# First four pairs' quotient with tokens in partitions: one denominator a token, turned back by TensorE into the first chunk's input

## The chip, the cores and the metric

One core of a Trainium2 chip runs the kernel. The metric is the device time of one execution in microseconds (us); of the kernel before, three runs gave 948.98, 949.53 and 950.82, so the median is 949.53 us. TensorE does matrix products into PSUM, ScalarE (ACT) and VectorE (DVE) do the element-wise work, GpSimd (POOL) does element-wise work between SBUF tiles, and SyncE (SP) issues most of the loads.

## The reference

```python
def phi(x):                                        # x: q or k, times D ** -0.25
    proj = np.einsum('bhsd,md->bhsm', x, omega)
    h = proj - np.sum(x * x, axis=-1, keepdims=True) / 2.0
    return np.exp(h - np.max(h, axis=-1, keepdims=True)) / np.sqrt(m)
kv = np.einsum('bhsm,bhsd->bhmd', k_p, v)
z = np.sum(k_p, axis=2)
num = np.einsum('bhsm,bhmd->bhsd', q_p, kv)
den = np.einsum('bhsm,bhm->bhs', q_p, z)[..., None] + 1e-06
attn_out = num / den
...
h = x @ w_in;  g = h * np.clip(h + 3.0, 0.0, 6.0) / 6.0;  x = g @ w_out
h = x @ w_in2; g = h / (1.0 + np.exp(-1.702 * h));        out = g @ w_out2
```

There are 4 batches of 8 heads with 576 tokens and head size 64, 128 features, and two layers of width 512 with 2048 hidden units over the 2304 tokens. All is float32. The denominator is one number for each token and head.

## The kernel before

The 32 heads are taken as 16 pairs. A pair fills the 128 partitions with two heads' 64 dimensions, and its 576 tokens are four tiles of 128 and a tail of 64 (`ST`, `TAIL`). The five first pairs (`LEAD` = 5, numbers 0 to 4) are computed in a first stage, since the first chunk of 512 tokens of the layers needs four pairs (`PPB` = 4, one batch). Chunk 0 then starts, and the other eleven pairs are spread by a table of slots (`slot_units`) through the layers' products, where TensorE always has work.

For a pair the steps are these. `projection` (L479, L486) makes the features' exponents in PSUM. VectorE takes the row maxima (L866, L863) and from them and the norms two small operations (L878, L881: `h_max` and `bias`), `statistics` in all, once each for queries, keys and tail. ScalarE takes the exponentials (L685, L679). TensorE turns the queries' tiles (`turn`, L506) and ScalarE copies them out (L691), so that features lie in partitions. `key_values` (L516 to L522) multiplies keys with the values and a column of ones. VectorE copies the result into `state` (`keep`, L899 to L901); the sum of the keys is spread there over 64 columns. `numerator` (L542 in pairs 0 to 3, L553 later) then gives numerators and denominators with dimensions in partitions, in halves of 288 tokens. ScalarE copies the denominators out (L695), VectorE takes their reciprocal (L906) and multiplies (L910) into `X`.

The layers run in float32r with a high and a low part of every operand: ScalarE rounds `X` to `x_hi` (L739) and the low part `x_lo` is the difference, by GpSimd for the first three pairs (L398) and by VectorE for the fourth (L930). `hidden` (L585, L586, L591) makes the hidden blocks and `output` (L610 to L612) the second product. Block 0 of chunk 0 is done in four parts, one for each pair, inside the first stage; the layers' unbroken work begins with hidden block 1. GpSimd rounds and splits the first three pairs of weight blocks (`early_high` L412, `early_part` L403) and folds the squared rows of pairs 2 to 4 into norms (`fold_rows`, L378 and L380), all in the first stage. ScalarE squares the rows (L668).

Each engine has its own program in one fixed order, written out by hand at the ends of the engine blocks; engines wait for one another by counting semaphores. PSUM has eight banks: four for the projections of queries and keys (`acc`), one for hidden blocks and tails, and three (`att`) for turning, key-values and numerators.

## Time and profile before

| | before |
|---|---|
| median of three runs | 949.53 us |
| the profiled execution | 950.23 us |
| its span, first to last instruction | 947.9 us |
| TensorE busy | 934.7 us (99%) |
| VectorE busy | 402.7 us (42%) |
| ScalarE busy | 383.5 us (40%) |
| GpSimd busy | 174.1 us (18%) |

The span is the profiled execution without 2.3 us around it. TensorE is busy nearly all the time, so the end moves when TensorE's work changes, when it gets its work later, or when its clock changes. The shares are means over a first stage and the long remainder, and are to be read stage by stage.

### The profile page before, as it was taken

The numbers are of one execution on the slowest core, as the hardware profiler recorded it, in microseconds if no ns is written. First come the engines' busy times: TensorE is split into PE (matmuls) and PEld (weight loads), VectorE is DVE, ScalarE is ACT, GpSimd is POOL, SyncE is SP. The second block draws the span as 40 slices with busy tenths as digits, with TensorE's granted clock in tenths as the row PEclk, the third lists the DMA queues.
The fourth block names the chain that finished last, engine by engine and source line by source line (L and its number), as shares of the span: only waits on it lengthen the run. The fifth ranks groups of instructions, "written<-read, shape, count | busy, mean of one in ns | idle before, by whom it ended". The sixth has DMA issues, their size and how long they took to land.

```text
span 947.9 us, 12947 instructions
## 1 busy us (share of the span) xinstructions
PE 934.7 (99%) x5098; PEld 778.4 (82%) x5098; DVE 402.7 (42%) x708; ACT 383.5 (40%) x879; POOL 174.1 (18%) x185
## 2 busy tenths in 40 slices
PE   8899999999999999999999999999999999999998
PEld 6668788878888778888889988888888888888898
DVE  6866655655446553452223442233223222422332
ACT  7756555554445544442225652232223222322322
POOL 2575566121221120000004830000000000000000
PEclk9999999999999999999999999999999999999999
DMA  9434442111121211010002610001001000100010
GB/s 279 124 94 133 124 133 63 57 45 39 50 63 39 63 26 38 1 45 0 1 1 82 179 52 1 1 1 45 1 1 45 1 0 1 45 1 1 5 41 23
DMA packets 40731, 45.98 MB, mean 49 GB/s; under 512 B 21600, under 2 KB 22240, under 8 KB 40672
## 3 DMA queue, kind: packets, MB, share of 16 engines
q1 hardware_dynamic: 40304, 44.54, 15.6%
q8 instruction: 40, 0.66, 0.3%
q10 hardware_dynamic: 368, 0.62, 0.2%
q14 instruction: 19, 0.16, 0.1%
HBM read 40.44 MB, written 4.72 MB: 48 GB/s over the span
## 4 chain that ended last, share of the span: by engine, by line
PE 94%; DVE 4%; ACT 1%; issue 0%; DVEq 0%
PE acc L610 14%; PE acc L611 14%; PE acc L612 14%; PE hid L585 11%; PE hid L591 10%; PE hid L586 10%; PE att L585 4%; PE att L586 4%; PE att L591 4%; PE att L486 3%; PE att L553 2%; PE att L522 2%; PE att L506 1%; DVE row_max L866 1%; PE att L479 1%; DVE k_phi_b L906 1%
## 5 line engine op out<-in xcount | busy, mean ns | idle before, releaser
L610 PE MATMUL acc<-g_hi,w_out_hi 128*128 128x512 f32 (+1 forms) x640 | 241.5, 377 | 0.0
L612 PE MATMUL acc<-g_hi,w_out_lo 128*128 128x512 f32 (+1 forms) x640 | 236.0, 369 | 0.0
L611 PE MATMUL acc<-g_lo,w_out_hi 128*128 128x512 f32 (+1 forms) x640 | 235.9, 369 | 0.0
L585 PE MATMUL hid<-x_hi,w_in_hi 128*128 128x512 f32 (+1 forms) x476 | 181.7, 382 | 1.7 <-ACT x_hi L739 1.7
L591 PE MATMUL hid<-x_lo,w_in_hi 128*128 128x512 f32 (+1 forms) x476 | 176.2, 370 | 0.3 <-DVE x_lo L930 0.3
L586 PE MATMUL hid<-x_hi,w_in_lo 128*128 128x512 f32 (+1 forms) x476 | 175.5, 369 | 0.0
L945 DVE TENSOR_TENSOR g_lo<-R,g_hi 128x512 fp32r<-128x512 f32 (+1 forms) x160 | 106.9, 668 | 91.0 <-ACT g_hi L756 91.0
L610 PEld LDWEIGHTS acc<-g_hi,w_out_hi 128*128 128x128 f32 x640 | 120.8, 189 | 21.3 <-issue 1.9
L612 PEld LDWEIGHTS acc<-g_hi,w_out_lo 128*128 128x128 f32 x640 | 120.7, 189 | 20.5
L611 PEld LDWEIGHTS acc<-g_lo,w_out_hi 128*128 128x128 f32 x640 | 120.8, 189 | 19.3
L756 ACT ACTIVATE g_hi<-R 128x512 fp32r<-128x512 f32 (+1 forms) x160 | 94.6, 591 | 85.7 <-DVE R L940 52.6
L585 PEld LDWEIGHTS hid<-x_hi,w_in_hi 128*128 128x128 f32 x476 | 89.8, 189 | 19.7 <-issue 2.3
L938 DVE SCALAR_TENSOR_TENSOR R<-R,hid 128x512 f32<-128x512 f32 (+1 forms) x79 | 49.9, 631 | 129.2 <-ACT R L747 129.2
L591 PEld LDWEIGHTS hid<-x_lo,w_in_hi 128*128 128x128 f32 x476 | 89.7, 188 | 16.8 <-DVE x_lo L930 1.1
L586 PEld LDWEIGHTS hid<-x_hi,w_in_lo 128*128 128x128 f32 x476 | 89.9, 189 | 14.3
L747 ACT ACTIVATE R<-hid 128x512 f32<-128x512 f32 (+1 forms) x79 | 43.9, 556 | 106.0 <-PE hid L591 105.9
L940 DVE TENSOR_TENSOR R<-R,hid 128x512 f32<-128x512 f32 (+1 forms) x40 | 25.4, 634 | 113.5 <-ACT R L749 113.5
L940 DVE TENSOR_TENSOR R<-R,att 128x512 f32<-128x512 f32 (+1 forms) x40 | 25.4, 634 | 113.0 <-ACT R L749 113.0
L906 DVE RECIPROCAL k_phi<-k_phi 128x288 f32<-128x288 f32 x28 | 54.5, 1948 | 38.9 <-ACT k_phi L702 38.9
L749 ACT ACTIVATE R<-att 128x512 f32<-128x512 f32 (+1 forms) x40 | 22.2, 555 | 116.9 <-PE att L591 116.4
L749 ACT ACTIVATE R<-hid 128x512 f32<-128x512 f32 (+1 forms) x40 | 22.2, 555 | 116.2 <-PE hid L591 116.2
L585 PE MATMUL att<-x_hi,w_in_hi 128*128 128x512 f32 (+1 forms) x164 | 61.1, 372 | 0.0
(132 smaller groups left out, 1044.8 us busy)
## 6 DMA issues: line engine op xcount, KB each, us to landing
X<-w_in SPq DMA_DIRECT2D x16, 256.0 KB, 2.6
X<-w_out SPq DMA_DIRECT2D x16, 256.0 KB, 2.8
out_t<-X SPq DMA_DIRECT2D x16, 256.0 KB, 2.3
q_cols<-q_t SPq DMA_DIRECT2D x14, 288.0 KB, 2.8
k_cols<-k_t SPq DMA_DIRECT2D x14, 288.0 KB, 3.3
rows<-q_n SPq DMA_DIRECT2D x13, 288.0 KB, 3.5
rows<-k_n SPq DMA_DIRECT2D x13, 288.0 KB, 3.1
v_rows<-v_n SPq DMA_DIRECT2D x14, 256.0 KB, 3.3
```

Source lines behind the costliest of these rows:

```text
L585: nc.tensor.matmul(bank, w_hi[0][:, at], x_hi[:, k, x0:x0 + t], start=(k == 0), stop=False)
L586: nc.tensor.matmul(bank, w_lo[0][:, at], x_hi[:, k, x0:x0 + t], start=False, stop=False)
L591: last = nc.tensor.matmul(bank, w_hi[0][:, at], x_lo[:, k, x0:x0 + t], start=False, stop=(k == KC - 1))
L610: nc.tensor.matmul(bank, w_hi[1][:, at], g_hi[:, g, 0:t], start=(s == 0), stop=False)
L611: nc.tensor.matmul(bank, w_hi[1][:, at], g_lo[:, g, 0:t], start=False, stop=False)
L612: last = nc.tensor.matmul(bank, w_lo[1][:, at], g_hi[:, g, 0:t], start=False, stop=(s == J - 1))
L749: nc.scalar.activation(R[:, 0:t], h, ACT.Sigmoid, scale=1.702).then_inc(gate_ready, 1)
L756: nc.scalar.activation(g_hi[:, n % G_SLOTS, 0:t], R[:, 0:t], ACT.Copy).then_inc(g_hi_ready, 1)
L906: nc.vector.reciprocal(d, d).then_inc(recip_done, 1)
L938: nc.vector.scalar_tensor_tensor(out=r, in0=r, scalar=6.0, in1=h, op0=ALU.min, op1=ALU.mult).then_inc(gated, 1)
L940: nc.vector.tensor_tensor(r, r, h, ALU.mult).then_inc(gated, 1)
L945: nc.vector.tensor_tensor(g_lo[:, n % G_SLOTS, 0:t], R[:, 0:t], g_hi[:, n % G_SLOTS, 0:t].bitcast(F32), ALU.subtract).then_inc(g_ready, 1)
```

## The change

In pairs 0 to 3 the quotient is computed with tokens in partitions. `keep` copies key-values and the keys' sum as they are, 65 columns for a head. `quotient` on TensorE uses the turned queries as the stationary operand and these 65 columns as the moving one, once for a tile of 128 tokens and head, and the tail's tile against both heads. The 65th column is the denominator. VectorE adds the epsilon to nine columns of denominators, takes one reciprocal of 128x9, and multiplies by it into a tile by tokens (`xs`, named x_by_token). TensorE turns that back (`turn_back`), four tiles and the tail. ScalarE rounds the four tiles from PSUM straight to `x_hi`; VectorE copies only the tail's 64 tokens to `X` and takes `x_lo` from PSUM. The denominators' copies on ScalarE, the copies by halves, and GpSimd's three `x_lo` go. Two of ScalarE's squares come earlier, the others after the turned queries. GpSimd folds and splits in another order. The diff, cut to its core:

```diff
@@ keep @@
-                if by_columns(a):
-                    ones, values = state[:, 2:4, :], state[:, 0:2, :]
...
+                if by_token(a):
+                    nc.vector.tensor_copy(state[:].rearrange("p c d -> p (c d)")[:, 0:2 * (D + 1)],
+                                          bank[:, P:P + 2 * (D + 1)]).then_inc(state_ready, 1)
+                    nc.vector.tensor_copy(tile_of(a, KQ, 0, ST), bank[:, 0:P]).then_inc(tails_out, 1)
+                    return
@@ TensorE @@
+            def quotient(a):
+
+                q, sums = q_turned(a), state[:].rearrange("p c d -> p (c d)")[:, 0:2 * (D + 1)]
...
+                if a > 0:
+                    pe.wait_ge(x_ready, a)
+                for h in range(2):
+                    for t in range(ST):
+                        last = nc.tensor.matmul(num_bank(a, h)[:, t * (D + 1):(t + 1) * (D + 1)], q[:, h, t * P:(t + 1) * P],
+                                                sums[:, h * (D + 1):(h + 1) * (D + 1)], start=True, stop=True)
+                    if h == 0:
+                        last = nc.tensor.matmul(num_bank(a, 0)[:, ST * (D + 1):(ST + 2) * (D + 1)], tile_of(a, KQ, 0, ST), sums,
+                                                start=True, stop=True)
+                    last.then_inc(nd_done, 2)
+
+            def turn_back(a):
+                pe.wait_ge(xs_ready, a + 1)
+                for t in range(ST):
+                    nc.tensor.transpose(back_bank(a)[:, t * P:(t + 1) * P], xs[:, t, :], ident[:])
+                nc.tensor.transpose(num_bank(a, 0)[:, 0:P], xs[:, ST, :], ident[:]).then_inc(xs_turned, 1)
@@ turn @@
                 if 0 < a < LEAD and h == 0:
-                    pe.wait_ge(den_ready, dens_to(a - 1, 1))
+                    pe.wait_ge(xs_ready, a)
                 elif 0 < a < LEAD:
-                    pe.wait_ge(x_written, 2 * (a - 1) + 1)
+                    pe.wait_ge(x_written, 2 * (a - 1) + 2)
@@ ScalarE @@
+            def first_high(a):
+
+                act.wait_ge(xs_turned, a + 1)
+                nc.scalar.activation(x_hi[:, a, 0:ST * P], back_bank(a)[:, 0:ST * P], ACT.Copy).then_inc(x_hi_ready, 1)
@@ VectorE @@
+            def quotient(a):
+                tiles = [num_bank(a, h)[:, 0:ST * (D + 1)].rearrange("p (t c) -> p t c", t=ST) for h in range(2)]
+                dve.wait_ge(nd_done, 4 * a + 2)
+                nc.vector.tensor_scalar(dens[:, 0:ST], tiles[0][:, :, D], EPS, None, ALU.add)
+                for h in range(2):
+                    rows_h, _, den = tail_of(h)
+                    nc.vector.tensor_scalar(dens[rows_h, 2 * ST:GROUPS], num_bank(a, 0)[rows_h, den], EPS, None, ALU.add)
+                dve.wait_ge(nd_done, 4 * a + 4)
+                nc.vector.tensor_scalar(dens[:, ST:2 * ST], tiles[1][:, :, D], EPS, None, ALU.add).then_inc(dens_set, 1)
+                dve.wait_ge(dens_set, a + 1)
+                nc.vector.reciprocal(dens[:], dens[:]).then_inc(dens_ready, 1)
...
+                    nc.vector.tensor_tensor(xs[:, 0:ST, h * D:(h + 1) * D], tiles[h][:, :, 0:D],
+                                            dens[:, h * ST:(h + 1) * ST].unsqueeze(2).to_broadcast([P, ST, D]), ALU.mult)
...
+            def take_back(a):
+
+                dve.wait_ge(xs_turned, a + 1)
+                for h in range(2):
+                    rows_h = slice(h * D, (h + 1) * D)
+                    nc.vector.tensor_copy(x_at(a, ST * P, TAIL, h * D, (h + 1) * D), num_bank(a, 0)[rows_h, rows_h]).then_inc(x_written, 1)
+                dve.wait_ge(x_hi_ready, a + 1)
+                nc.vector.tensor_tensor(x_lo[:, a, 0:ST * P], back_bank(a)[:, 0:ST * P], x_hi[:, a, 0:ST * P].bitcast(F32),
+                                        ALU.subtract).then_inc(x_ready, 1)
@@ order of VectorE @@
                 keep(a)
                 statistics(a + 1, "k")
                 statistics(a + 1, "tail")
-                normalise(a, 0)
-                normalise(a, 1)
-                if a + 2 < LEAD - 1:
-                    statistics(a + 2, "q")
+                quotient(a)
+                statistics(a + 2, "q")
+                take_back(a)
@@ order of GpSimd @@
+            for a in (2, 3, 4):
+                fold_rows(a)
+                for r in (2 * a - 4, 2 * a - 3):
+                    early_high(r)
+                    early_part(r)
```

On TensorE the part from the numerators of pair 1 to the key-values of pair 2 stands in the kernel before as follows (`att` and `acc` are PSUM banks, `hid` the bank of the tails):

```order
L542 MATMUL att<-q_phi_b,state 64x288 x4
L486 MATMUL acc<-omega,X 128x128 x8
L542 MATMUL att<-q_phi_b,state 64x288 x4
L506 MATMUL att<-ident,q_phi 128x128 x4
L486 MATMUL acc<-omega,X 128x128 x8
L506 MATMUL att<-ident,q_phi 128x128 x4
L516 MATMUL att<-ident,q_tail_phi 128x128
```

In the changed kernel TensorE has at the same place:

```order
L523 MATMUL att<-state,q_phi_b 128x65 x4
L526 MATMUL att<-state,q_tail_phi_b 128x130
L523 MATMUL att<-state,q_phi_b 128x65 x4
L475 MATMUL acc<-omega,X 128x128 x8
L495 MATMUL att<-ident,q_phi 128x128 x4
L533 MATMUL att<-ident,x_by_token 128x128 x4
L534 MATMUL att<-ident,x_by_token 128x128
L475 MATMUL acc<-omega,X 128x128 x8
L495 MATMUL att<-ident,q_phi 128x128 x4
L503 MATMUL att<-ident,q_tail_phi 128x128
```

The second half of the quotient now stands ahead of the next projection, and five turns back stand between the two turns of the next pair's queries.

VectorE has, from the tail's statistics to the copy of the next pair's key-values, in the kernel before:

```order
L881 SCALAR_TENSOR_TENSOR bias<-h_max,half_norm 128x2
L906 RECIPROCAL k_phi_b<-k_phi_b 128x288
L910 TENSOR_TENSOR X<-att,k_phi_b 128x288
L906 RECIPROCAL k_phi_b<-k_phi_b 128x288
L910 TENSOR_TENSOR X<-att,k_phi_b 128x288
L866 TENSOR_REDUCE row_max<-acc 128x4 x2
L878 SCALAR_TENSOR_TENSOR h_max<-row_max,half_norm 128x8
L881 SCALAR_TENSOR_TENSOR bias<-h_max,half_norm 128x8
L899 COPY state<-att 128x128
```

and in the changed kernel:

```order
L899 TENSOR_SCALAR dens<-att 128x4
L902 TENSOR_SCALAR dens<-att 64x1 x2
L904 TENSOR_SCALAR dens<-att 128x4
L906 RECIPROCAL dens<-dens 128x9
L912 TENSOR_TENSOR x_by_token<-att,dens 128x4x64
L914 TENSOR_TENSOR x_by_token<-att,dens 64x64
L912 TENSOR_TENSOR x_by_token<-att,dens 128x4x64
L914 TENSOR_TENSOR x_by_token<-att,dens 64x64
L850 TENSOR_REDUCE row_max<-acc 128x4 x2
L865 SCALAR_TENSOR_TENSOR h_max<-row_max,half_norm 128x8
L868 SCALAR_TENSOR_TENSOR bias<-h_max,half_norm 128x8
L923 COPY X<-att 64x64 x2
```

The statistics of the next queries (L850 to L868) now stand between the quotient and the copies out of the turned-back tail; `x_lo` (L925) follows the copies.

GpSimd has in the kernel before, from the fold of pair 3 to that of pair 4:

```order
L378 TENSOR_TENSOR X<-X 128x18x32
L378 TENSOR_TENSOR X<-X 128x18x16
L378 TENSOR_TENSOR X<-X 128x18x8
L378 TENSOR_TENSOR X<-X 128x18x4
L378 TENSOR_TENSOR X<-X 128x18x2
L380 TENSOR_TENSOR half_norm<-X 128x18
L403 TENSOR_TENSOR w_out_lo<-X,w_out_hi 128x512
L412 CAST w_in_hi<-X 128x512
L412 CAST w_out_hi<-X 128x512
```

and in the changed kernel, for pair 2 and again for 3 and 4:

```order
L390 TENSOR_TENSOR rows<-rows 128x18x32
L390 TENSOR_TENSOR rows<-rows 128x18x16
L390 TENSOR_TENSOR rows<-rows 128x18x8
L390 TENSOR_TENSOR rows<-rows 128x18x4
L390 TENSOR_TENSOR rows<-rows 128x18x2
L392 TENSOR_TENSOR half_norm<-rows 128x18
L419 CAST w_in_hi<-X 128x512
L410 TENSOR_TENSOR w_in_lo<-X,w_in_hi 128x512
L419 CAST w_out_hi<-X 128x512
L410 TENSOR_TENSOR w_out_lo<-X,w_out_hi 128x512
```

Four operations on weights now stand behind every fold. In the kernel before, four stood ahead of the first fold, three behind each of the first two, and three `x_lo` and two more behind the last.

## Rows read from the trace of the kernel before

**Rows 1.** Windows: us, busy (count) of PE, PEld, DVE, ACT, POOL, PEclk, DMA, GB/s.

```profile
0.00:57.63 57.63, 47.63 (x418) 35.99 (x418) 45.14 (x99) 39.39 (x114) 25.81 (x39) 0.99 0.62 186
57.63:947.90 890.27, 887.05 (x4682) 742.37 (x4680) 357.58 (x610) 344.08 (x765) 148.32 (x146) 1.00 0.13 40
```

**Rows 2.** Timeline, VectorE, pair 2: start, length in us, line, output<-input, count.

```profile
37.58 0.28 DVE L899 COPY state<-att 128x128 f32<-128x128 f32 x1
...
38.18 1.28 DVE L866 TENSOR_REDUCE row_max<-acc 128x4 f32<-128x512 f32 x2
...
39.85 0.42 DVE L863 TENSOR_REDUCE row_max<-hid 128x2 f32<-128x256 f32 x1
...
40.65 1.95 DVE L906 RECIPROCAL k_phi<-k_phi 128x288 f32<-128x288 f32 x1
42.70 0.46 DVE L910 TENSOR_TENSOR X<-att,k_phi 128x288 f32<-128x288 f32 x1
43.07 1.95 DVE L906 RECIPROCAL k_phi<-k_phi 128x288 f32<-128x288 f32 x1
...
47.68 0.29 DVE L899 COPY state<-att 128x128 f32<-128x128 f32 x1 [2.10 <-PE att L522]
```

**Rows 3.** Timeline, TensorE, pair 2.

```profile
33.72 1.16 PE L486 MATMUL acc<-omega,X 64*128 64x128 f32 x16 [0.41 <-ACT k_phi L685]
34.82 0.66 PE L506 MATMUL att<-ident,q_phi 128*128 128x128 f32 x4
35.31 0.27 PE L516 MATMUL att<-ident,q_tail_phi 128*128 128x128 f32 x1
...
37.47 0.65 PE L479 MATMUL hid<-omega,X 64*64 64x128 f32 x8
```

**Rows 4.** Timeline, VectorE: a narrow reciprocal and product.

```profile
55.72 0.55 DVE L915 RECIPROCAL k_phi_b<-k_phi_b 128x64 f32<-128x64 f32 x1
56.30 0.23 DVE L917 TENSOR_TENSOR X<-att,k_phi_b 128x64 f32<-128x64 f32 x1
```

**Rows 5.** Timeline, TensorE, products 1, 7 and 13 from hidden block 1 on.

```profile
57.63 0.79 PE L585 MATMUL att<-x_hi,w_in_hi 128*128 128x512 f32 x1
...
60.30 0.40 PE L585 MATMUL att<-x_hi,w_in_hi 128*128 128x512 f32 x1
...
61.67 0.39 PE L610 MATMUL acc<-g_hi,w_out_hi 128*128 128x512 f32 x1
```

**Rows 6.** Windows around the drop of TensorE's clock, columns as in rows 1.

```profile
53.50:56.90 3.40, 1.41 (x8) 0.74 (x9) 3.17 (x7) 1.86 (x4) 0.37 (x1) 0.99 0.51 154
56.90:60.30 3.40, 3.40 (x14) 2.55 (x11) 2.42 (x8) 2.16 (x9) 0.62 (x1) 0.51 0.44 140
```

**Rows 7.** Timeline, VectorE: pair 0's copy, and two small operations.

```profile
16.83 0.29 DVE L899 COPY state<-att 128x128 f32<-128x128 f32 x1
...
19.02 1.15 DVE L881 SCALAR_TENSOR_TENSOR bias<-h_max,half_norm 128x8 f32<-128x8 f32 x1
...
37.14 0.52 DVE L881 SCALAR_TENSOR_TENSOR bias<-h_max,half_norm 128x8 f32<-128x8 f32 x1
```

**Rows 8.** Timeline, GpSimd.

```profile
16.28 0.61 POOL L412 CAST w_in_hi<-X 128x512 fp32r<-128x512 f32 x1 [14.81 <-DVE bias L881]
...
18.88 1.27 POOL L403 TENSOR_TENSOR w_out_lo<-X,w_out_hi 128x512 fp32r<-128x512 f32 x1
...
31.35 3.59 POOL L378 TENSOR_TENSOR X<-X 128x576 f32<-128x576 f32 x5 [4.02 <-ACT X L668]
...
35.27 1.27 POOL L403 TENSOR_TENSOR w_out_lo<-X,w_out_hi 128x512 fp32r<-128x512 f32 x1
...
37.03 0.61 POOL L412 CAST w_out_hi<-X 128x512 fp32r<-128x512 f32 x1
```

**Rows 9.** Timeline, ScalarE, a copy of turned queries, and squares.

```profile
35.51 0.60 ACT L691 ACTIVATE q_phi<-att 128x512 f32<-128x512 f32 x1 [0.93 <-PE att L506]
...
40.00 1.31 ACT L668 ACTIVATE rows<-rows 128x576 f32<-128x576 f32 x2
```

More of the change, by code:

```diff
@@ L193, in groups, with by_token @@
             return t[:, :, 2 * ST] if u == "tail" else t[:, (KQ, KK)[u == "k"], 0:2 * ST]
-        def by_columns(a):
+        def by_token(a):
             return a < LEAD - 1
         def three(a):
-            return (att[0], att[2], att[1]) if a < LEAD and a % 2 else (att[2], att[0], att[1])
+            return tuple(att[(1 + min(a, LEAD - 1) + i) % 3] for i in range(3))
         def proj_banks(a, u):
@@ L214, in kv_bank, with num_bank, back_bank @@
         def kv_bank(a):
-            return three(a)[0 if by_columns(a) else 2]
-        def den_bank(a, half):
-            return three(a)[2 - half]
-        def num_bank(a, half):
-            return three(a)[2 * half]
+            return three(a)[0 if by_token(a) else 2]
+        def num_bank(a, h):
+            return three(a)[2 - h]
+        def back_bank(a):
+            return three(a)[0]
         def head_bank(a, half, h):
@@ L226, in dens_to @@
         def dens_to(a, half, h=1):
-            return 2 * a + half + 1 if by_columns(a) else 2 * (LEAD - 1) + 4 * (a - LEAD + 1) + 2 * half + h + 1
+            return 4 * (a - LEAD + 1) + 2 * half + h + 1
         def tile_of(a, kind, h, t):
@@ L628, in _ @@
             projection(1, "k")
-            for a in range(LEAD - 1):
+            for a in range(LEAD - 2):
                 key_values(a)
-                if a + 1 < LEAD - 1:
-                    projection(a + 1, "tail")
-                else:
-                    hidden(0, (0,))
-                numerator(a, 0)
-                if a + 1 == LEAD - 1:
-                    hidden(0, (1,))
-                if a + 2 < LEAD:
-                    projection(a + 2, "q")
-                numerator(a, 1)
-                if a + 2 < LEAD:
-                    turn(a + 1, 0)
-                    projection(a + 2, "k")
-                    turn(a + 1, 1)
-            hidden(0, (2,))
+                projection(a + 1, "tail")
+                quotient(a)
+                projection(a + 2, "q")
+                turn(a + 1, 0)
+                turn_back(a)
+                projection(a + 2, "k")
+                turn(a + 1, 1)
+            key_values(LEAD - 2)
+            hidden(0, (0,))
+            quotient(LEAD - 2)
+            hidden(0, (1,))
+            turn_back(LEAD - 2)
             turn(LEAD - 1, 0)
             turn(LEAD - 1, 1)
-            hidden(0, (3,))
+            hidden(0, (2, 3))
             projection(LEAD - 1, "tail")
@@ L674, in exps @@
                     act.wait_ge(nd_done, 4 * before + 4)
-                if u != "q" and before >= 0:
+                if u != "q" and 0 <= before < LEAD - 1:
+                    act.wait_ge(kv_done, before + 1)
+                elif u != "q" and before >= 0:
                     act.wait_ge(x_written, 2 * before + 2)
@@ new lines, in take_back @@
+            def take_back(a):
+                dve.wait_ge(xs_turned, a + 1)
+                for h in range(2):
+                    rows_h = slice(h * D, (h + 1) * D)
[3 more added lines that the diff above has]
+                                        ALU.subtract).then_inc(x_ready, 1)
```

184 lines of the change are left out of this document (71 added, 113 removed).

## The prediction

> **What bounds the kernel now.** I read the page's busy shares first, then windows over the whole run, then the first stage's timelines engine by engine. The windows split the run at 57.63 us, where hidden block 1 begins [rows 1]. Behind it TensorE is busy 887.05 of 890.27 us, and the change leaves that work as it is, so nothing is won there except by TensorE's clock. Ahead of it TensorE is busy 47.63 of 57.63 us, and VectorE 45.14. So the question is at what time the changed kernel starts hidden block 1.
>
> Inside the first stage the pairs follow at a fixed distance. VectorE's copy of the key-values, which I call T, starts at 37.58 for pair 2 and 47.68 for pair 3, 10.10 us apart [rows 2]; it starts at 16.83 for pair 0 [rows 7]. A reciprocal of 288 columns takes 1.95 us and there are two in a pair, from 40.65 on, each followed by a product of 0.37 us before the next starts [rows 2]. VectorE waits for nothing there, but ahead of 47.68 it sat idle 2.10 us for TensorE: the queries' statistics no longer stand in that turn.
>
> **The change, part by part.** I follow one pair from T to the next T. Behind the two projections and the numerators TensorE has a wait in its program for the quotient in the tile by tokens; that wait is what ends last, so the loop is VectorE to the quotient, and TensorE from there.
>
> VectorE, from T. `keep` is two copies and not three; three take 38.18 - 37.58 = 0.60 us, so 0.40. The statistics of keys and tail are unchanged, 40.65 - 38.18 = 2.47 [rows 2]. The quotient so starts at T + 2.87. Its first operations have no row. The four additions on at most four columns cost at least the 0.07 that the narrowest copy would if only its fixed part (0.20 less 128 columns at one a nanosecond) were left, and at most the 0.20 of a whole copy [rows 2]. They are nearest to that fixed part, so 0.10, 0.40 in all. The reciprocal of 9 columns follows from 1.95 us for 288 [rows 2] and 0.55 for 64 [rows 4]: 0.00625 a column and 0.15 fixed, 0.21. Waits on its own results cost 0.10 each, as between the reciprocal's end at 42.60 and the product at 42.70 [rows 2]; there are two. A product of 256 columns is 0.37 less 32 columns, 0.34; one of 64 columns 0.23 long with its end under the next one, 0.15 [rows 4]; two of each are 0.98. The strided and spread operands have no row: between nothing and, if they halved the rate, another 0.65. I take nothing, since the copies and reductions from PSUM run at one column a nanosecond too. The quotient is 0.40 + 0.21 + 0.20 + 0.98 = 1.79 us, in place of about 4.8. It is ready at T + 4.66.
>
> To that comes GpSimd. VectorE's small operations on two SBUF operands, h_max and bias, normally take 0.17 us, but one took 1.15 and ended at 20.17, when GpSimd's w_out_lo of 18.88 + 1.27 ended, and another 0.52 to 37.66, when a cast of 37.03 + 0.61 ended [rows 7, 8]. GpSimd's fold now runs beside the keys' statistics in every pair: for the locks on its short pieces I add 0.25 (between 0 and 0.6). So T + 4.91.
>
> The Trainium skill, "SBUF — State Buffer", section "SBUF: two separate sides", says that a VectorE operation with two SBUF inputs and a GpSimd operation exclude each other for a whole instruction. This trace agrees with 20.17 against 20.15. By the rule the sum keeps the 0.25 and the rival below stands; if only the rate were shared, both would be near nothing.
>
> TensorE from there: 0.12 to see the signal (an estimate, since such gaps in the trace are hidden in the idle time; 0.05 to 0.2). Four turns are 35.31 - 34.82 = 0.49; the five turns back at the same rate 0.61; the keys' projection 34.82 - 33.72 = 1.10; then the second four turns and the key-values, 37.58 - 34.82 = 2.76 up to the next copy [rows 2, 3]. That is 5.08. The next T is at T + 9.99, 0.11 less than before. So most of the 3 us that VectorE saves ends as idle time on it: what is late next is TensorE's own chain, with five turns back added and all of it behind the quotient.
>
> The quotient's nine products are as many and as wide as the nine of key_values, which take 37.47 - 35.31 - 0.12 = 2.04 us [rows 3]. They run from T + 0.45 on under VectorE's statistics, and the queries' projection behind them too, so they cost nothing; if the statistics were gone, T + 2.5 would be the bound. ScalarE loses two denominators' copies, and rounds x_hi as before, one in each pair; it is busy 39.39 of 57.63 us [rows 1]. Its squares of pair 2 come ahead of exponentials that nothing on the path waits for. GpSimd loses three x_lo; VectorE takes them on, behind the copies, in its idle time. SP's loads of rows wait for folds that come no later than before.
>
> Three periods from 16.83 give T of pair 3 at 46.80 in place of 47.68. Then the end of the stage, with no statistics ahead of the quotient. One part of hidden block 0 (three products at 1.37 / 6 = 0.23, 0.69) [rows 5] starts 0.04 ahead of T; the nine products end at T + 2.69; VectorE needs 0.03 + 0.10 + 0.20 + 0.21 + 0.98 = 1.52 behind them, T + 4.21; signal and five turns back 0.73, T + 4.94; first four turns, T + 5.43, under which the two tail copies pass; second four, T + 5.92; two parts of block 0, 1.37, T + 7.29; the tail's projection of pair 4, 0.65 [rows 3], T + 7.94. Hidden block 1 starts at 46.80 + 7.94 = 54.74 and not 57.63: 2.89 us earlier. Before, TensorE waited for four reciprocals and products in this stretch; that is where most of the gain lies.
>
> The clock. Between 53.50 and 56.90 TensorE was busy 1.41 of 3.40 us, and from 56.90 to 60.30 its granted clock was 0.51, the level of 1.2 GHz [rows 6]. Six products of hidden block 1 took 60.30 - 57.63 = 2.67 us; the next six, at the level of 2.4, 61.67 - 60.30 = 1.37 [rows 5]. The new end of the stage has one idle time of 1.5 us and is else dense, so I expect no drop: 1.30 less.
>
> One thing decides between cases. GpSimd's chain starts when ScalarE's squares end. These follow the copy of the second turned block: T - 2.76 + 0.49 + 0.60 + 1.31 [rows 9] puts the fold's start near T - 0.3. It takes 35.27 - 31.35 = 3.92, and w_out_lo starts 18.88 - 16.28 = 2.60 behind the fold [rows 8]: near T + 6.2, to T + 7.5. The queries' h_max comes after the quotient and the two maxima, at T + 4.91 + 1.4 = T + 6.3, and its copies must be out when TensorE wants the second four turns, at T + 7.23. A hit moves h_max to T + 7.5, bias and copies to T + 8.0 and TensorE to T + 8.1: 0.9 us for that pair. The two times are within what I know, so each of three pairs may be hit; I take one, 0.9.
>
> Sum: 2.89 + 1.30 - 0.90 = 3.29 us less. The profiled execution's 950.23 us would be 946.9; from the median of 949.53, 946.2 us.
>
> **The rivals.**
> 1. GpSimd hits every pair. For it: the chains of both engines hang on the same TensorE block, so that what happens in one pair repeats in the next. Against it: 0.1 us decides. Three hits cost 2.7: 2.89 + 1.30 - 2.7 = 1.5 less, 948.0. None costs 0: 4.19 less, 945.3.
> 2. The clock falls once in the new stage as well, somewhere, since each pair has a wait of some 1.4 us on TensorE, one longer than the 0.41 before the keys' projection now [rows 3]. The 1.30 is then not won: 947.5.
> 3. Slower: the clock falls in every pair. Place: between the queries' projection and the turns, in all four pairs. Price: one spell costs 1.30 on solid products; four and the old one kept cost 5.2 against 2.89 - 0.90 = 2.0 won, 3.2 more, 952.7. It decides from the second spell on. Against it: from pair to pair TensorE would stay busy some 8 of 10 us, near the share of the whole first stage before, in which it fell only behind 1.41 of 3.40.
> 4. The change doesn't do what it says: the strided reads at half rate, 0.65 on each quotient, four times, 2.6 us; with a hit 948.8, no change to be seen.
>
> **How the numbers follow.** The forecast with none or one hit 0.45; two or three hits 0.27; one new drop 0.12; slow reads 0.06; slower 0.10. A measurement of this kernel can't tell less than 0.2%, 1.9 us. Faster than 947.6: 0.43 of the forecast, 0.12 of the hits (two give 947.1), 0.07 of the one drop: 0.62. Slower than 951.4: 0.10. Between: 0.28. The range goes from the case without hits and with the low bounds of additions and locks (1.1 more, 944.2) to the slow reads, 949.2.
>
> **What would show it.** In the changed kernel's timeline: copies of state 10.0 us apart, or 10.9 with a hit; a quotient of about 1.8 us on VectorE; an h_max or bias of the queries over 0.5 us beside w_out_lo is a hit; hidden block 1 near 55.6; granted clock 1.00 from there on. An interval over 11 us, a clock under 1 inside the pairs, or an idle TensorE behind hidden block 1 would make the prediction wrong.

## The result, and the profile after

| | before | changed |
|---|---|---|
| median | 950.1 us (20 runs, 947.7 to 950.8) | 950.92 us (20 runs, 950.0 to 953.1) |
| ratio of the two, 95% interval | | 1.0015, 1.0008 to 1.0022 |
| profiled execution, its span | 950.23, 947.9 us | 951.39, 948.6 us |
| state copies (T) of pairs 0 to 3 | 16.83, 27.47, 37.58, 47.68 | 16.88, 28.97, 39.92, 50.85 |
| hidden block 1 starts | 57.63 | 59.26 |
| from there to the end of the span | 890.27 | 889.34 |

The forecast was 946.2 us, 3.3 less than the 949.53 it started from. The changed kernel is 0.15% slower than before by the ratio, less than the 0.2% that I called no change. Hidden block 1 starts 1.63 us later and not 2.89 earlier; what follows it is 0.93 us shorter. The difference of the spans is the sum, 0.70.

Two things stand in the times of the single executions, each of which has its span and its mean granted clock on record. First, what lies outside the span grew: its median is 2.34 us in the 93 executions of the kernel before that ran beside the experiments (2.27 to 2.41) and 2.80 in the 20 of the changed kernel (2.71 to 2.92). That is 0.46 of the 0.8 us between the medians, and its cause is open. Second, the mean clock tells whether it fell: it is 0.998 in the profiled executions of both kernels, each with one fall, and 1.000 in one without. It was 0.998 or less in 71 of the 93 executions before (median 950.39 us; the other 22: 948.90) and in 11 of the 20 of the changed kernel (951.39; the other nine: 950.65). Without a fall the changed kernel is 1.75 us slower, not 0.8.

The page's line of busy times for the changed kernel:

```profile
PE 935.4 (99%) x5126; PEld 784.9 (83%) x5126; DVE 398.7 (42%) x734; ACT 380.8 (40%) x871; POOL 170.1 (18%) x182
```

VectorE and GpSimd are each 4.0 us less busy, ScalarE 2.7 (before: 402.7, 174.1, 383.5). The removed work is gone, and the time did not follow. Windows of the changed kernel, in the columns of [rows 1]: split at hidden block 1, then a stretch in pair 0, then the two stretches of [rows 6].

```profile
0.00:59.26 59.26, 49.45 (x447) 43.44 (x447) 38.75 (x124) 36.80 (x106) 22.15 (x36) 0.97 0.59 181
59.26:948.60 889.34, 885.98 (x4682) 741.44 (x4680) 359.98 (x610) 344.02 (x766) 147.96 (x146) 1.00 0.13 40
...
22.40:26.00 3.60, 3.60 (x25) 3.27 (x25) 3.31 (x7) 1.20 (x2) 2.10 (x3) 0.53 0.97 329
...
53.50:56.90 3.40, 2.27 (x16) 1.58 (x15) 2.10 (x9) 0.81 (x2) 0.00 (x0) 1.00 0.00 0
56.90:60.30 3.40, 3.40 (x23) 2.51 (x22) 2.94 (x7) 1.65 (x4) 0.00 (x0) 1.00 0.00 0
```

Against [rows 1], VectorE is busy 38.75 us in the first stage where it was 45.14, 6.4 less, and the stage is longer all the same. (Behind it VectorE is busy 2.4 us more in this execution; in e11 below it is busy 396.6 us in all, so that this part doesn't repeat.) Against [rows 6], the clock stays at 1.00 at the end of the stage, as forecast. It fell in another place, to 0.53 in pair 0.

VectorE in pair 2 of the changed kernel, which answers to [rows 2] (start, length, line, output<-input, count, and in brackets the idle time ahead and what ended it):

```profile
39.92 0.29 DVE L883 COPY state<-att 128x130 f32<-128x130 f32 x1 [2.16 <-PE att L509]
...
41.71 0.25 DVE L865 SCALAR_TENSOR_TENSOR h_max<-row_max,half_norm 128x8 f32<-128x8 f32 x1
...
42.61 0.35 DVE L865 SCALAR_TENSOR_TENSOR h_max<-row_max,half_norm 128x2 f32<-128x2 f32 x1
...
43.07 0.16 DVE L899 TENSOR_SCALAR dens<-att 128x4 f32<-128x4 f32 x1
43.14 0.32 DVE L902 TENSOR_SCALAR dens<-att 64x1 f32<-64x1 f32 x2
43.48 0.16 DVE L904 TENSOR_SCALAR dens<-att 128x4 f32<-128x4 f32 x1
43.67 0.22 DVE L906 RECIPROCAL dens<-dens 128x9 f32<-128x9 f32 x1
43.92 0.42 DVE L912 TENSOR_TENSOR x_by_token<-att,dens 128x256 f32<-128x256 f32 x1
44.26 0.20 DVE L914 TENSOR_TENSOR x_by_token<-att,dens 64x64 f32<-64x64 f32 x1
44.39 0.41 DVE L912 TENSOR_TENSOR x_by_token<-att,dens 128x256 f32<-128x256 f32 x1
44.81 0.23 DVE L914 TENSOR_TENSOR x_by_token<-att,dens 64x64 f32<-64x64 f32 x1
45.07 1.29 DVE L850 TENSOR_REDUCE row_max<-acc 128x4 f32<-128x512 f32 x2
46.47 0.92 DVE L865 SCALAR_TENSOR_TENSOR h_max<-row_max,half_norm 128x8 f32<-128x8 f32 x1
47.42 0.17 DVE L868 SCALAR_TENSOR_TENSOR bias<-h_max,half_norm 128x8 f32<-128x8 f32 x1
47.50 0.47 DVE L923 COPY X<-att 64x64 f32<-64x64 f32 x2
```

GpSimd and TensorE beside it:

```profile
46.09 1.27 POOL L410 TENSOR_TENSOR w_out_lo<-X,w_out_hi 128x512 fp32r<-128x512 f32 x1
```

```profile
45.19 0.63 PE L495 MATMUL att<-ident,q_phi_b 128*128 128x128 f32 x4 [1.39 <-DVE x_by_token L914]
45.65 0.60 PE L533 MATMUL att<-ident,x_by_token 128*128 128x128 f32 x4
46.09 0.27 PE L534 MATMUL att<-ident,x_by_token 128*128 128x128 f32 x1
46.29 1.16 PE L475 MATMUL acc<-omega,k_cols 64*128 64x128 f32 x16
48.12 0.63 PE L495 MATMUL att<-ident,q_phi_b 128*128 128x128 f32 x4 [0.66 <-DVE X L923]
```

The queries' h_max takes 0.92 and not 0.17 us, and ends at 47.39, 0.03 behind w_out_lo's 47.36. Behind it in VectorE's order stand bias and the tail's two copies to X; TensorE, with the keys' projection done, waits 0.66 us for them. This is the hit of my prediction. It occurs in all three pairs: the same h_max takes 0.92 at 23.68, 1.11 at 35.34 and 0.92 at 46.47.

### The profile page after: what moved, and what is told of

Same layout as the page of the kernel before. It is cut to its first block, busy times and chain, and to the rows that moved or that the text cites. A ratio compares the mean times of both kernels' runs of the same rounds, so it can differ in the third digit from the quotient of the medians.

```text
span 948.6 us, 12977 instructions
## 1 busy us (share of the span) xinstructions
PE 935.4 (99%) x5126; PEld 784.9 (83%) x5126; DVE 398.7 (42%) x734; ACT 380.8 (40%) x871; POOL 170.1 (18%) x182
## 2 busy tenths in 40 slices
DMA packets 40731, 45.99 MB, mean 48 GB/s; under 512 B 21600, under 2 KB 22240, under 8 KB 40672
## 4 chain that ended last, share of the span: by engine, by line
PE 96%; DVE 3%; ACT 0%; issue 0%; DVEq 0%
PE acc L604 14%; PE acc L606 14%; PE acc L605 14%; PE hid L581 11%; PE hid L585 10%; PE hid L582 10%; PE att L581 4%; PE att L585 4%; PE att L582 4%; PE att L509 3%; PE att L475 3%; PE att L549 2%; PE att L495 1%; DVE row_max L850 1%; PE att L468 1%; DVE h_max L865 0%
## 5 line engine op out<-in xcount | busy, mean ns | idle before, releaser
L961 DVE TENSOR_TENSOR g_lo<-R,g_hi 128x512 fp32r<-128x512 f32 (+1 forms) x160 | 110.8, 692 | 91.5 <-ACT g_hi L750 91.5
L931 DVE RECIPROCAL k_phi<-k_phi 128x288 f32<-128x288 f32 x24 | 46.8, 1950 | 37.5 <-ACT k_phi L696 37.5
```

The lines of the kernel that those rows point to most:

```text
L931: nc.vector.reciprocal(d, d).then_inc(recip_done, 1)
L961: nc.vector.tensor_tensor(g_lo[:, n % G_SLOTS, 0:t], R[:, 0:t], g_hi[:, n % G_SLOTS, 0:t].bitcast(F32), ALU.subtract).then_inc(g_ready, 1)
```

## The experiments

Ratios are against the kernel before on the same chip. Unless said otherwise an experiment is the changed kernel with the edit shown. "Hidden block 1" is its start in the profiled execution. It carries the place of pair 0's T with it, which moves by up to 1.04 us between profiled executions. So the stretch from there to hidden block 1 compares them better: 40.80 us before, 41.45 in e11 and 42.38 in the changed kernel's profiled execution, with its fall of the clock. A "fall" counted in executions is a mean granted clock of 0.998 or less.

**e11_changed_again: the changed kernel, unedited.** It asks which of the things seen in one trace repeat.

> The changed kernel once more, unedited, to see which of its features repeat. Theory A (the hits by GpSimd repeat in every execution, the fall of the clock in pair 0 is chance): TensorE waits again for the tail's copies ahead of the second turns of pairs 2 and 3, 0.5 to 1 us each; in pair 0 either the clock is at 1.00 and there is such a wait of 0.5 to 0.9 us too, or it is lower and there is none. Theory B (the fall of the clock is fixed by the program): granted clock under 0.8 again between 20 and 26.5 us. Median 950.9, within 0.5 us, in either case.

Measured: 951.00 us, ratio 1.0007 (0.9999 to 1.0016); T 17.15, 28.33, 39.26, 50.19; hidden block 1 at 58.60. Its windows over the first stage and over pair 0:

```profile
0.00:58.60 58.60, 48.24 (x446) 42.58 (x446) 38.72 (x124) 36.74 (x106) 22.13 (x36) 1.00 0.60 183
...
20.00:26.50 6.50, 4.20 (x50) 3.71 (x50) 5.70 (x18) 3.76 (x13) 4.45 (x8) 1.00 1.03 321
```

The three hits repeat (h_max 0.93, 0.92, 0.93 us), the clock's fall in pair 0 doesn't, though TensorE waits 1.63 us there and waited 1.64 in the other. So the hits belong to the kernel and the fall is a matter of chance (4 of these 11 executions have one); it costs the trace of the changed kernel 0.91 us (first spacing 12.09 against 11.18).

**e1_late_split and e5_tail_first: two ways to take the hit away.** The first keeps GpSimd's second split back until the queries' bias is out; the second moves the tail's copies ahead of h_max on VectorE, so that only h_max is held up.

```diff
@@ e1, GpSimd, early_part @@
+                    if r % 2:
+                        pool.wait_ge(bias_ready, 3 * a + 1)
@@ e5, VectorE @@
-                statistics(a + 2, "q")
+                maxima(a + 2, "q")
+                take_tail(a)
+                biases(a + 2, "q")
                 take_back(a)
...
```

> The changed kernel, but GpSimd's second split of each round (w_out_lo) waits until VectorE's bias of the next queries is out, so the two can't exclude each other. Theory A (GpSimd holds up h_max, and with it the copies that TensorE waits for): no h_max of the queries over 0.3 us; TensorE's waits ahead of the second turns of pairs 2 and 3 (0.86 and 0.66 us) go; hidden block 1 starts 1.5 us earlier, near 57.8, and the kernel takes 1.5 us less than the changed one. Theory B (the long h_max comes from something else, or the wait is covered by TensorE's other work): nothing moves by more than 0.3 us.

> The changed kernel with another order on VectorE alone: the next queries' maxima, then the copies out of the turned-back tail, then h_max and bias of the queries, then x_lo. GpSimd is as in the changed kernel. Theory A (what costs is that the copies stand behind an h_max that GpSimd holds up): h_max stays long, up to 1 us, but TensorE's waits of 0.86 and 0.66 us go, and hidden block 1 starts near 57.8, 1.5 us earlier. Theory B (TensorE would wait as long for another thing): under 0.5 us is won.

Measured: e1 949.07 us, ratio 0.9989 (0.9980 to 0.9997), T 16.45, 26.92, 37.15, 47.38, hidden block 1 at 55.78. e5 948.86 us, 0.9990 (0.9981 to 0.9999), T 16.33, 26.80, 37.02, 47.24, hidden block 1 at 55.64. VectorE and GpSimd in pair 2 of e5:

```profile
43.49 0.48 DVE L923 COPY X<-att 64x64 f32<-64x64 f32 x2
44.00 0.48 DVE L865 SCALAR_TENSOR_TENSOR h_max<-row_max,half_norm 128x8 f32<-128x8 f32 x1
```

```profile
43.19 1.27 POOL L410 TENSOR_TENSOR w_out_lo<-X,w_out_hi 128x512 fp32r<-128x512 f32 x1
```

TensorE in the same pair:

```profile
43.39 1.16 PE L475 MATMUL acc<-omega,k_cols 64*128 64x128 f32 x16
44.48 0.66 PE L495 MATMUL att<-ident,q_phi_b 128*128 128x128 f32 x4
```

The copies from PSUM run at their usual 0.23 each while w_out_lo is under way; h_max, two SBUF operands, is held until 44.48, 0.02 behind w_out_lo's end. The wait of 0.66 is gone and the turns follow the projection at once. The two edits touch different engines and both give spacings of 10.22 or 10.23 for pairs 1 and 2 where e11 has 10.93, and hidden block 1 near 55.7 where e11 has 58.60. Of these 2.9 us 0.7 to 0.8 are the place of pair 0's T; from there to hidden block 1 it is 39.33 and 39.31 us against 41.45, so 2.1 for three hits. The cause of the hits and their price are shown. The rule of the Trainium skill that the prediction cited ("SBUF — State Buffer", section "SBUF: two separate sides") speaks of VectorE operations with two SBUF inputs only; these rows agree with it, in that the copies, whose source is in PSUM, are left alone.

**e2_fill and e3_both: is it the clock?** Four identity products stand in TensorE's idle time before the first turns, in the changed kernel (e2) and in e1 (e3).

```diff
+                fill(4, back_bank(a))
                 turn(a + 1, 0)
```

> The changed kernel with four products of the identity with itself in each of pairs 0 to 2, between the queries' projection and the turns, into a bank that is free there; their result is never read. TensorE idles 1.64 us there in pair 0 and 1.2 to 1.4 in the others. Theory A (the clock falls in pair 0 since TensorE idles): the granted clock stays 1.00 between 20 and 26.5 us in place of 0.74; the keys' projection takes 1.16 and not 1.95 us; the second turns then wait for the copies, until about 25.3, so hidden block 1 starts 0.9 us earlier, near 58.4. Theory B (the clock falls for narrow products, not for idling): the clock falls as before, and the products cost 0 to 0.3 us.

> Both earlier edits of the changed kernel together: GpSimd's second split waits for the queries' bias, and four products of the identity stand in TensorE's idle time of pairs 0 to 2. With the late split alone hidden block 1 began at 55.78 us and the clock happened not to fall in the profiled execution. Theory A (the clock falls by chance in some executions where TensorE idles 1.4 to 1.6 us; filling prevents it): hidden block 1 within 0.3 us of 55.8, and a median 0.3 to 0.8 us under the late split's 949.1. Theory B (the clock has no part in the median): the same median as with the late split alone, within 0.3 us.

Measured: e2 950.34 us, ratio 1.0004 (0.9995 to 1.0014), clock 1.00 in the first stage, waits for X of 0.68, 0.67 and 0.68, hidden block 1 at 58.01. e3 948.12 us, 0.9982 (0.9973 to 0.9991), hidden block 1 at 56.48. Fill alone leaves the hits where they were (from pair 0's T to hidden block 1 41.45 us, as in e11); its median is 0.6 us below the unedited kernel's 950.92, and the intervals overlap. With the hits gone, fill takes 0.95 off the median (949.07 to 948.12, intervals overlapping again), though the stretch to hidden block 1 is the same in the profiled executions (39.32, e1 39.33). What it takes away is falls: 6 of e1's 11 executions have one, and 1 of e3's; those without one have medians of 947.96 and 948.06. Of e2's 11 none has one. Without the fill, taking the hits away was worth 1.9 us (950.92 to 949.07; by the ratios 1.7 to 2.5): the clock is the smaller part.

**e4_before_fill: the kernel before with its clock held up.** Six identity products ahead of the last part of hidden block 0, in the kernel before.

```diff
+            fill(6, acc[0])
```

> The kernel before, with six products of the identity with itself between pair 4's turns and the last part of hidden block 0, where TensorE idles 1.68 us; their result is never read. Theory A (that idle time lets the clock fall from 56.9 to 60.3): the granted clock stays 1.00, the first six products of hidden block 1 take 1.37 and not 2.67 us, and the kernel takes 1.3 to 1.6 us less than the kernel before. Theory B (the idle time isn't what decides): the clock falls there all the same and the time stays.

Measured: 949.40 us, ratio 0.9997 (0.9988 to 1.0006). Its windows:

```profile
57.74:946.80 889.06, 885.72 (x4682) 741.51 (x4680) 357.63 (x612) 343.75 (x765) 147.85 (x146) 1.00 0.13 40
53.50:56.90 3.40, 3.02 (x20) 2.17 (x18) 3.16 (x6) 1.73 (x4) 0.85 (x1) 1.00 0.58 154
```

From hidden block 1 to the end of the span it takes 889.06 us against 890.27 [rows 1]: 1.2 us of the 1.30 that I gave the clock, in this one trace. In the medians the gain can't be told from none. The clock of the kernel before doesn't fall in every execution: 24 of the 32 beside e4 have a fall, and 2 of e4's 11, so the fill does prevent most of them. But the executions of e4 without one have a median of 949.2, and those of the kernel before 948.7; why is open. The 1.30 is the worth of the fall where it occurs, not of the median: over all 93 executions those with and without a fall are 1.5 us apart.

**e7_old_gpsimd: GpSimd's order of before in the changed kernel.**

```diff
-            for a in (2, 3, 4):
-                fold_rows(a)
-                for r in (2 * a - 4, 2 * a - 3):
-                    early_high(r)
-                    early_part(r)
+            pool.wait_ge(bias_ready, 4)
+            for r in (0, 1):
+                early_high(r)
+                early_part(r)
+            fold_rows(2)
...
```

> The changed kernel with GpSimd's folds and splits in the order of the kernel before (two casts next to one another, splits apart, four weight operations ahead of the first fold); all else as changed. Theory A (the new order on GpSimd is what puts a split on the queries' h_max): in pairs 1 and 2 TensorE's waits of 0.86 and 0.66 us shrink under 0.3, in pair 0 one operation of VectorE is held up by over 1 us as before the change; hidden block 1 starts near 57, 2 us ahead of the changed kernel's 59.26. Theory B (any order of GpSimd's work hits as often): within 0.7 us of 59.26.

Measured: 952.78 us, ratio 1.0033 (1.0020 to 1.0045); T 17.17, 31.71, 41.88, 51.97; hidden block 1 at 60.37. Two operations of VectorE in pair 0, and the window on TensorE behind them:

```profile
20.55 1.32 DVE L878 SCALAR_TENSOR_TENSOR bias<-h_max,half_norm 128x2 f32<-128x2 f32 x1
...
25.46 1.20 DVE L878 SCALAR_TENSOR_TENSOR bias<-h_max,half_norm 128x8 f32<-128x8 f32 x1
```

```profile
23.90 1.09 PE L505 MATMUL att<-ident,q_phi_b 128*128 128x128 f32 x4 [2.85 <-DVE x_by_token L924]
```

```profile
24.00:27.00 3.00, 3.00 (x17) 2.67 (x19) 2.83 (x6) 1.20 (x2) 2.56 (x5) 0.50 0.79 248
27.00:30.00 3.00, 3.00 (x21) 2.78 (x19) 0.75 (x2) 0.85 (x2) 0.00 (x0) 0.50 0.68 246
```

Pairs 1 and 2 have no hit and are 10.17 and 10.09 apart. Pair 0 takes 14.54: its tail's bias and its queries' bias are held up for 1.15 and 1.03 us, TensorE idles 2.85, and the clock then stands at 0.50 for six us; the mean clock is 0.996 or less in all five executions. So theory A holds for pairs 1 and 2 and fails for the total, 60.37 and not 57: it had allowed one hold-up in pair 0, and there are two and the clock. The new order of GpSimd's work was needed, for pair 0; it moved the collision to the queries' h_max of every pair.

**e6_keys_early and e8_end_too: TensorE's order.** With the hits gone TensorE still waits 1.38 to 1.64 us a pair for the quotient. e6 is e5 with the keys' projection and the turns back ahead of the turns, so that the wait comes earlier and the tail's copies have cover; ScalarE rounds x_hi ahead of both its copies of turned queries. e8 is e6 with three products more ahead of the last turns back.

```diff
@@ e6 @@
-                turn(a + 1, 0)
-                turn_back(a)
...
+                turn_back(a)
+                turn(a + 1, 0)
@@ e8, the end of the stage, on top @@
-            hidden(0, (1,))
+            hidden(0, (1, 2))
...
-            hidden(0, (2, 3))
+            hidden(0, (3,))
```

> The changed kernel with the tail's copies first on VectorE (as in the run before), and with another order on TensorE: the next keys' projection (1.1 us) ahead of the turns, where TensorE idles for the quotient, then the turns back, then both turns; ScalarE rounds x_hi ahead of both copies of turned queries. Theory A (TensorE's chain behind the quotient sets the distance of pairs, 10.2 us now): the distance falls to 9.4 to 9.8 us and hidden block 1 starts 1.2 to 2.0 us ahead of 55.64. Theory B (what is won on TensorE is lost on waits for the keys' exponentials and for the tail's copies): 10.0 to 10.3 us, within 0.5 us of 55.64.

> The order with the keys' projection early, and at the stage's end the third part of hidden block 0 (0.69 us) moved ahead of the last turns back, where TensorE idles 0.92 us. Theory A (that idle time is real slack): hidden block 1 starts 0.6 to 0.7 us ahead of the run with the keys' projection early alone. Theory B (x_hi, the turned queries' copies or block 0's end come late instead, and TensorE waits behind): under 0.2 us.

Measured: e6 948.09 us, ratio 0.9982 (0.9973 to 0.9990), state copies 10.26, 10.22 and 10.22 apart, hidden block 1 at 55.99. e8 947.33 us, 0.9972 (0.9961 to 0.9983), hidden block 1 at 55.56. TensorE in pair 2 of e8:

```profile
42.42 1.16 PE L475 MATMUL acc<-omega,k_cols 64*128 64x128 f32 x16 [0.93 <-ACT k_phi_b L678]
43.52 0.66 PE L533 MATMUL att<-ident,x_by_token 128*128 128x128 f32 x4
```

The quotient is no longer waited for, and the spacing is the same 10.22. What is waited for now is the keys' exponentials, since their bank must be read before the next projection; they start behind the keys' statistics on VectorE. That is another chain of nearly the same length, so e6's own expectation of a shorter pair fell. e8's held: from pair 3's T to hidden block 1 it takes 7.72 us, e6 8.42. Both medians are below e5's, with narrower spreads (947.6 to 948.9 and 947.0 to 947.8, e5 947.6 to 950.2). The longest idle time in a pair is 0.98 now, and none of their 18 executions has a fall of the clock; 2 of e5's 11 have. That narrows the spread but is not all of it: e5's nine without a fall have a median of 948.8 and e6's eleven 948.1. The stretch from pair 0's T is 0.19 shorter in e6 (39.12, e5 39.31); the rest is open.

**e10_stats_alone and e9_keys_stats_first: the keys' statistics ahead of keep.** VectorE idles 2.15 us before keep (2.10 before [rows 2]), and the statistics of the next keys could stand there. e10 does it in the changed kernel for pairs 1 to 3, e9 on top of e8.

```diff
+                if a > 0:
+                    dve.wait_ge(exp_done, banks_to(a, "k", 1))
+                    statistics(a + 1, "k")
                 keep(a)
-                statistics(a + 1, "k")
+                if a == 0:
+                    statistics(a + 1, "k")
...
```

> The changed kernel with that one edit alone: the next keys' statistics ahead of keep on VectorE in pairs 1 to 3. Theory A (in the changed kernel TensorE idles ahead of the first turns since the quotient comes behind the keys' statistics): the idle time of 1.2 to 1.4 us ahead of the turns of pairs 2 and 3 falls under 0.6 us, and hidden block 1 starts 1 to 3 us ahead of 59.26. It may also move the queries' h_max off GpSimd's last split, since it comes 1 us earlier, and so take one or two of the hits away. Theory B: GpSimd's splits meet it all the same, and under 0.7 us is won.

> The version with all orders changed so far (tail's copies first, keys' projection early, hidden block 0's third part early), and on VectorE the next keys' statistics (1.67 us) ahead of keep in pairs 1 to 3, in the 2.2 us in which VectorE waits for the key-values; GpSimd as in the changed kernel. Theory A (the distance of pairs is set by the statistics that stand between keep and the keys' exponentials and the quotient): the distance of pairs 1 and 2 falls from 10.2 us to 8.7 to 9.3, hidden block 1 starts 1.5 to 3 us ahead of 55.56, the median is near 945. Theory B (another chain, of about 10 us, lies just behind, such as ScalarE's or the row folds): over 9.9 us, within 0.7 us of 55.56.

Measured: e10 948.23 us, ratio 0.9980 (0.9971 to 0.9988); T 17.33, 28.52, 38.09, 47.64; hidden block 1 at 56.05. e9 949.57 us, 0.9986 (0.9973 to 0.9998), in two heaps, four executions at 946.5 to 946.8 and eight at 948.9 to 950.4. VectorE in pair 2 of e10:

```profile
37.24 0.17 DVE L865 SCALAR_TENSOR_TENSOR h_max<-row_max,half_norm 128x8 f32<-128x8 f32 x1
...
38.09 0.29 DVE L883 COPY state<-att 128x130 f32<-128x130 f32 x1 [0.48 <-PE att L509]
```

The idle time falls from 2.15 to 0.48 and pairs 1 and 2 from 10.93 to 9.57 and 9.55. Of these 1.37 us 0.67 is the hit, which goes from both pairs since h_max now comes ahead of w_out_lo (pair 0 keeps its own), and 0.72 is TensorE's wait for the quotient, 1.38 in e11 and 0.66 here, a little over the 0.6 expected. That second part is the saving of VectorE, collected. In e9's profiled execution it went wrong in one pair:

```profile
26.73 1.34 DVE L865 SCALAR_TENSOR_TENSOR h_max<-row_max,half_norm 128x8 f32<-128x8 f32 x1
28.11 0.17 DVE L868 SCALAR_TENSOR_TENSOR bias<-h_max,half_norm 128x8 f32<-128x8 f32 x1
28.19 0.29 DVE L883 COPY state<-att 128x130 f32<-128x130 f32 x1
```

```profile
28.78 1.65 PE L523 MATMUL att<-state,q_phi_b 128*128 128x65 f32 x8 [1.16 <-DVE state L883]
```

```profile
28.00:32.00 4.00, 3.22 (x17) 3.25 (x17) 1.92 (x10) 3.21 (x13) 3.53 (x8) 0.64 0.68 160
32.00:36.00 4.00, 4.00 (x35) 3.86 (x34) 2.77 (x8) 0.00 (x0) 2.26 (x3) 0.51 0.57 160
```

The early h_max met GpSimd's fold, whose first piece ran from 26.65 to 28.05, keep stood behind it, TensorE idled 1.16 us, and the clock fell: T 12.24 apart, and hidden block 1 at 57.97 where 1.5 to 3 us ahead of 55.56 was expected. The two heaps are falls that come or don't: the four short executions have mean clocks of 0.999 and 1.000, of the eight long ones two have 0.998 (948.9 and 949.1) and six, with the profiled one, 0.996 (950.1 to 950.4).

**e12_one_pair_early: the best of it.** e8, three fill products between the projections in pairs 0 and 1, and the early statistics for the last pair alone.

```diff
+                if a < 2:
+                    fill(3, back_bank(a))
...
+                if a == 2:
+                    dve.wait_ge(exp_done, banks_to(a, "k", 1))
+                    statistics(a + 1, "k")
                 keep(a)
-                statistics(a + 1, "k")
+                if a < 2:
+                    statistics(a + 1, "k")
```

> On top of e8_end_too: three fill products (identity by identity, results never read) between the queries' and the keys' projection in pairs 0 and 1, where TensorE stood idle 0.93 to 0.97 us for the keys' exponentials, and the next keys' statistics ahead of the keep copy in pair 2 alone. Theory A (the statistics shorten a pair wherever GpSimd does not hold them up, and the fill keeps the clock steady): state copies 10.2 and 10.2 apart, then 8.8 to 9.2; end stage 7.7 us as in e8_end_too; hidden block 1 at 53.9 to 54.3 instead of 55.56; clock 1.00; median 945.7 to 946.6. Theory B (the early statistics of the last pair are held up by GpSimd's split, or another chain takes over): hidden block 1 within 0.5 us of 55.56 and the median within 0.4 us of e8_end_too's 947.3.

Measured: 946.51 us (945.4 to 947.8 in five executions, none with a fall), ratio 0.9966 (0.9952 to 0.9979); T 16.30, 26.58, 36.79, 45.99; hidden block 1 at 53.69, a little ahead of what theory A gave. Its windows, and h_max and GpSimd in pair 2:

```profile
0.00:53.69 53.69, 49.61 (x459) 43.05 (x459) 37.96 (x122) 36.63 (x106) 22.12 (x36) 1.00 0.66 200
53.69:943.00 889.31, 886.00 (x4682) 741.43 (x4680) 358.02 (x613) 344.29 (x766) 147.50 (x146) 1.00 0.13 40
```

```profile
42.46 0.47 DVE L930 COPY X<-att 64x64 f32<-64x64 f32 x2
42.97 1.13 DVE L872 SCALAR_TENSOR_TENSOR h_max<-row_max,half_norm 128x8 f32<-128x8 f32 x1
```

```profile
42.81 1.27 POOL L410 TENSOR_TENSOR w_out_lo<-X,w_out_hi 128x512 fp32r<-128x512 f32 x1
```

The last period is 9.20. The h_max is held up here too, to 44.10, by a w_out_lo from 42.81 to 44.08. It costs TensorE nothing: the copies that TensorE waits for are out ahead of it. TensorE is busy 49.61 of 53.69 us before hidden block 1. Hidden block 1 owes some of that to an early T in pair 0: from there it takes 37.39 us, e8 38.45. This version beats both kernels: 3.7 us less than before.

## Why the prediction was wrong

The step that failed is "I take one": the hit was allowed once in three pairs, and it comes every time. That was rival 1, to which I gave 0.27 together with two hits. The reason stood under that rival: GpSimd's chain and VectorE's hang on the same block of TensorE, so their distance is the same in every pair. w_out_lo starts 6.17 us behind T in pair 2 and 6.19 in pair 1, and h_max 6.55 and 6.37; I had put them at T + 6.2 and T + 6.3. The times were right to 0.3 us. Wrong was to make independent chances of what is one distance.

That step is the largest single one, but only a third of what the spans missed: 1.12 us, against 1.05 for the pairs' period, which was sized 0.27 too short in each, and 1.12 for the rest below. Rival 1's own time, 948.0, is still 2.9 under the measured 950.92. The recorded range ended at 949.2, for which its text gives only rival 4's 948.8; neither number holds the result.

Point by point, with the undisturbed trace of e11, where a clock at 1.00 leaves the steps bare:

- **The hits.** Three waits for the tail's copies, 0.67, 0.67 and 0.68: 2.02 us in place of the 0.90 charged, so 1.12 more. One costs less than 0.90, though it lasts as long as forecast (TensorE goes on at T + 8.20, 48.12 - 39.92, forecast 8.1): TensorE is through the keys' projection at T + 7.54 and not 7.23, so less of the time is waiting.
- **The pairs without hits.** e5's 10.22 against 9.99. From T to TensorE's next turn 5.26 (42.28 - 37.02) against 5.03, from there to the next T 4.96 against 4.96: TensorE's chain of turns, turns back, projection and key-values was right to the hundredth. The 0.12 for TensorE to see the quotient's signal was taken from no row; it was 0.15 (45.19 - 45.04). In the changed kernel's pair 2 the locks under GpSimd's fold cost 0.26 (h_max 0.25 and 0.35 for 0.17 each) against 0.25. The quotient took 1.97 (45.04 - 43.07) against 1.79: the additions with the wait behind them 0.60 for 0.50, the reciprocal with its wait 0.25 for 0.31, the products 1.12 for 0.98, of which 0.08 is the last one's end, which nothing overlaps. Pair 0 took 0.25 more, its keys' h_max being held for 0.51.
- **Where VectorE's 3 us went.** In pairs 0 and 1 into idle time before keep, 3.06 (with the clock's fall) and 2.16 us where there was none before, as forecast. In pair 2, where 2.10 us were idle already [rows 2], the queries' statistics of pair 4 took it, and 2.15 stay idle. e10 shows that a part could be had by moving the keys' statistics there: 0.72 us a pair.
- **The end of the stage.** T + 8.41 in place of 7.94. The tail's copies don't pass under the first four turns: TensorE waits 0.22 for them, in the changed kernel at 56.72. The turns back begin at T + 4.44 and not 4.33 (55.29 - 50.85), and the last two parts of block 0 take 1.57 and not 1.37 (58.67 - 57.10).
- **The clock.** The fall at the end of the stage [rows 6] is gone, and the part behind hidden block 1 is 0.93 to 0.97 us shorter (889.34, 889.30), not 1.30: 0.33 less won in e11. A fall comes in 71 of 93 executions of the kernel before and in 15 of 31 of the changed one, so the median wins less still. Rival 2, a fall inside a pair, came in the profiled execution and not in e11.
- **Rivals 3 and 4.** The clock doesn't fall in every pair (e11: 1.00 throughout). The strided reads don't run at half rate: a product of 256 columns took 0.42 with a start to start of 0.34 to the next, what I had taken for a plain one.

The sum closes for e11. Forecast for the span -3.29; the other hits +1.12; the periods +1.05 (0.27 in each of three, and pair 0's lock); end of the stage +0.47; T of pair 0 at 17.15 and not 16.83, +0.32; clock +0.33. That is 0.00, and both spans are 947.9. The changed kernel's profiled execution has 0.91 more for the clock in pair 0, 0.27 less at T of pair 0 and 0.06 in remainders: 948.6. That both spans are 947.9 is luck in part: T of pair 0 moves by more than its 0.32 from one execution to the next.

The median missed by more, 950.92 against 946.2: beside the 3.29 of the span there are the 0.46 outside it, which the prediction held fixed at 2.3, and 0.57 because the three first runs of the kernel before gave 949.53 and twenty give 950.1. Some 0.4 is left.

Not settled: what takes 0.46 us more outside the span, and why e5's median (948.86) lies 1.1 above its profiled execution (947.77), since only 2 of its 11 executions have a fall. For e1 (949.07 and 947.58) 6 of 11 have one, and the profiled one has none. Nor is it shown what decides whether the clock falls. T of pair 0 moved between 16.30 and 17.34 over the runs, for which no cause was looked for.

## What to carry to other kernels

When two engines' chains start from the same event, work out their distance once and price the collision for all iterations or for none. A hold-up costs what stands behind it in its engine's order: put the copies that the bottleneck waits for ahead of the operation that can be held up, as e5 and e12 do. Time saved on an engine becomes idle time in front of its next wait once another chain ends last, and is won only when work of the path, here the keys' statistics, is moved into it. Where executions of one kernel differ by a fall of the clock, compare those with it and those without it separately before reading a median.

## What the runs showed of the hardware

- Beside a train of GpSimd operations VectorE was let in after the one under way. In e7 the tail's bias began at 20.55 and ended at 21.87. The first of the fold's five pieces (576 columns) ran from 20.46 for 1.39 us, to 21.85, and the second (288 columns) began at 21.93. In e9 the first piece ended at 28.05 and h_max at 28.07.
- The same idle time doesn't always bring the same clock: behind 1.64 us of waiting in pair 0 the granted clock was 0.53 in the changed kernel's profiled execution, and behind 1.63 it was 1.00 in e11's. Identity products in TensorE's idle times made falls rare: none of e2's 11 executions has one and 1 of e3's, against 15 of 31 of the changed kernel and 6 of 11 of e1. At the lower level 16 products of the keys' projection took 1.95 us, at the higher 1.16.
- VectorE's smallest operations with a PSUM operand (4 columns, or 1 on 64 partitions) took 0.14 to 0.16 us each and followed each other in 0.07 to 0.18 us, where nothing had to be waited for.
